# Last stage in two passes over the tokens, with the up projection in seven block products in place of eight

## The chip, the cores and the metric

The kernel runs on one core of one Trainium2 chip. Its engines work from queues of their own and meet at semaphores: TensorE (PE) multiplies 128x128 stationary blocks with up to 512 moving columns and writes to PSUM (8 banks of 512 fp32 columns); VectorE (DVE), ScalarE (ACT) and GpSimd (POOL) work elementwise; SyncE (SP) issues most DMAs, POOL the loads of the weights. The metric is the device time of one execution in microseconds (us), lower is better.

## The reference

All arrays are fp32. A linear attention with decay gives x of 3072 tokens by 512 features; an MLP with gate (F = 1536) and an MLP with SoLU and layer norm (F2 = 1024) follow.

```python
state = gamma * state + k_t v_t^T;  y_t = scale * q_t state      # 4 batches, 8 heads, 768 tokens
x = y as (3072, 512)
xn = x / sqrt(mean(x * x) + 1e-06) * rms_g
act = silu(xn @ w_gate) * (xn @ w_val)                            # (3072, 1536)
x2 = act @ w_out                                                  # (3072, 512), "down"
h = x2 @ w_in                                                     # (3072, 1024), "up"
e = exp(h - max(h));  solu = h * e / (sum(e) + 1e-09)
ln = (solu - mean(solu)) / sqrt(var(solu) + 1e-06) * g_ln
out = ln @ w_out2                                                 # (3072, 512), "down2"
```

## The kernel before

Each fp32 operand a of a large product is split in two parts, high (a rounded to fp32r, made by ACT) and low (a - high, made by DVE), and a product is three matmuls: high high, low high, high low (`split_products`, L282). The first stage (attention and gate and value products, up to about 562 us) is not touched; it leaves act in DRAM (`act_dram`) and has most weights split by then.

The last stage goes once over six tiles of 512 tokens (`tiles`, `stage_c`). Per tile:
- **down** (`down`, L571): for each of 12 blocks k of F, 4 x 3 matmuls into the banks 0 to 3 (`DOWN`). SP loads act block k (`load_act`), ACT makes `act_hi` (`act_high`, L744), DVE `act_lo` (`act_low`, L984), and PE waits for that one before step k. Four buffers of `act_hi` let ACT run up to four steps ahead.
- the four sums x2 are split from the banks to `x2_hi`, `x2_lo` in SBUF.
- **up** (`up`, L589): for each of four blocks of 128 tokens and each half of F2 (512 columns), 4 slices x 3 matmuls into one of the two banks `H`. ACT copies h, DVE takes the maximum (`row_max`), ACT the exponent, DVE normalises and centres (`softmax_h`, `centre`).
- **turn** (L602): four transposes into the bank `TURN`, twice per token block; ACT and DVE split the turned block. **down2** (L612): 12 matmuls, twice per token block, into the bank `Y2`. ACT scales and SP stores.

The order on each engine is written out by hand: down steps of tile t have turn and down2 of blocks 2 and 3 of tile t - 1 between them, and up products those of blocks 0 and 1.

Weights come in 26 pieces of 128x1024 through a buffer of three slots, `w_raw`. POOL may load piece m once the low part of piece m - 3 is made (`load_weights`, L450). ACT and DVE split a piece as `weights_high` (L694) and `weights_low` (L930); w_out2's pieces are first scaled by g_ln on DVE (`scale_weights`). In tile 0 the four pieces of w_in (18 to 21) are split behind act blocks 4 to 7, two of w_out2 behind blocks 8 and 9, the last two (24, 25) behind the sums.

## Time and profile before

| | |
|---|---|
| three runs, us | 1046.56, 1046.72, 1050.99 (median 1046.72) |
| profiled execution | span 1048.8 us; its time is given by that span alone, 2.1 us over the median of the runs |
| PE busy | 1023.9 us, 98% |
| DVE, ACT, POOL busy | 460.4, 431.9, 90.4 us |
| last stage | from 562.61 us to the end |
| matmuls in the profile | 5496 |

The profile is of one execution. "Busy" is the time in which an engine has an instruction running; PE's matmuls overlap, so the mean duration of one is more than the time from one start to the next. `[0.50 <-DVE solu L1047]` behind a row says that the engine was idle for 0.50 us before it and what released it.

### The profile page before, as it was taken

How to read it: one execution, taken by the hardware profiler on the slowest of the kernel's cores; microseconds unless marked ns; L12 is line 12 of the kernel's file. 1: busy time of each engine (PE TensorE's matmuls, PEld its weight loads, DVE VectorE, ACT ScalarE, POOL GpSimd, SP SyncE). 2: the span in 40 equal slices, each digit the busy share in tenths (PEclk: the TensorE clock that was granted, in tenths of full speed). 3: DMA queues.
4: the chain of work that ended last, by engine and by line, in shares of the span. 5: the costliest groups of instructions: out<-in, count | busy, mean ns of one | idle time of the engine just before them, and what ended most of it. 6: DMA issues, size and time to landing. Idle time of an engine off the chain costs nothing.

```text
span 1048.8 us, 15480 instructions
## 1 busy us (share of the span) xinstructions
PE 1023.9 (98%) x5496; PEld 900.6 (86%) x5496; DVE 460.4 (44%) x874; ACT 431.9 (41%) x776; POOL 90.4 (9%) x101
## 2 busy tenths in 40 slices
PE   6799999999998999999999999999999999999998
PEld 4489999999998999999999888888888888888886
DVE  3847635356352463433324653253253254244243
ACT  3445333243231442413223464364364264265255
POOL 5321110111001011100000000000000000000000
PEclk9999999999999999999999999999999999999999
DMA  7664331532314234313134403013012012012000
GB/s 229 210 217 146 106 108 52 166 114 93 119 46 138 98 113 136 111 51 120 66 115 135 137 21 101 1 60 100 0 60 90 10 60 90 10 60 91 11 21 31
DMA packets 75656, 95.51 MB, mean 91 GB/s; under 512 B 7248, under 2 KB 59728, under 8 KB 75600
## 3 DMA queue, kind: packets, MB, share of 16 engines
q1 hardware_dynamic: 71856, 81.11, 24.1%
q0 software_dynamic: 3744, 13.63, 3.9%
q8 instruction: 38, 0.62, 0.3%
q14 instruction: 18, 0.15, 0.0%
HBM read 64.04 MB, written 30.67 MB: 90 GB/s over the span
## 4 chain that ended last, share of the span: by engine, by line
PE 93%; DVE 2%; DMA 1%; ACT 1%; issue 1%; SPq 0%; POOL 0%; DVEq 0%; ACTq 0%; POOLq 0%
PE psum L284 28%; PE psum L286 28%; PE psum L285 27%; PE psum L521 3%; PE psum L531 3%; PE psum L609 2%; PE psum L513 1%; DMA w_raw<-weights 1%; PE psum L548 1%; DMA v_buf<-v_rows 0%; PE psum L501 0%; DVE w_gv_lo L936 0%; ACT L802 0%; DMA chunk_decay_t<-chunk_decay 0%; DVE probs L897 0%
## 5 line engine op out<-in xcount | busy, mean ns | idle before, releaser
L284 PE MATMUL psum<-xn_hi,w_gv_hi 128*128 128x384 f32 x768 | 267.1, 348 | 1.0 <-issue 1.0
L286 PE MATMUL psum<-xn_hi,w_gv_lo 128*128 128x384 f32 x768 | 258.4, 336 | 2.6 <-issue 2.6
L285 PE MATMUL psum<-xn_lo,w_gv_hi 128*128 128x384 f32 x768 | 257.7, 336 | 0.0
L764 ACT ACTIVATE silu<-psum 128x384 f32<-128x384 f32 x96 | 47.2, 492 | 283.6 <-PE psum L286 283.6
L284 PEld LDWEIGHTS psum<-xn_hi,w_gv_hi 128*128 128x128 f32 x768 | 145.2, 189 | 4.3 <-issue 3.4
L286 PEld LDWEIGHTS psum<-xn_hi,w_gv_lo 128*128 128x128 f32 x768 | 144.9, 189 | 2.9 <-issue 2.9
L285 PEld LDWEIGHTS psum<-xn_lo,w_gv_hi 128*128 128x128 f32 x768 | 145.3, 189 | 0.9
L998 DVE TENSOR_TENSOR act_buf<-psum,silu 128x384 f32<-128x384 f32 x96 | 53.5, 557 | 199.9 <-PE psum L286 116.7
L284 PE MATMUL psum<-act_hi,w_out_hi 128*128 128x512 f32 x288 | 114.2, 397 | 0.0
L286 PE MATMUL psum<-act_hi,w_out_lo 128*128 128x512 f32 x288 | 112.3, 390 | 0.0
L285 PE MATMUL psum<-act_lo,w_out_hi 128*128 128x512 f32 x288 | 112.3, 390 | 0.0
L464 POOL TENSOR_TENSOR q_dec<-kq_buf,q_decay_t 64x384 f32<-64x384 f32 x64 | 72.5, 1132 | 317.8 <-PE psum L531 210.4
L284 PE MATMUL psum<-w_out_hi,ln_t_hi 128*128 128x512 f32 x192 | 76.3, 398 | 0.4 <-ACT out_buf L827 0.4
L284 PE MATMUL psum<-w_in_hi,x_hi 128*128 128x512 f32 x192 | 76.1, 396 | 0.0
L286 PE MATMUL psum<-w_in_hi,x_lo 128*128 128x512 f32 x192 | 74.9, 390 | 0.0
L286 PE MATMUL psum<-w_out_hi,ln_t_lo 128*128 128x512 f32 x192 | 74.9, 390 | 0.0
L285 PE MATMUL psum<-w_out_lo,ln_t_hi 128*128 128x512 f32 x192 | 74.9, 390 | 0.0
L285 PE MATMUL psum<-w_in_lo,x_hi 128*128 128x512 f32 x192 | 74.8, 390 | 0.0
L897 DVE TENSOR_TENSOR probs<-psum,mask_t 128x256 f32<-128x256 f32 x96 | 40.1, 417 | 74.5 <-PE psum L286 52.2
L986 DVE TENSOR_TENSOR act_lo<-act_raw,act_hi 128x512 fp32r<-128x512 f32 x72 | 48.2, 689 | 55.4 <-ACT act_hi L753 55.4
L1026 DVE TENSOR_REDUCE neg_max<-h_buf 128x1 f32<-128x1024 f32 x24 | 29.3, 1220 | 93.6 <-ACT h_buf L798 93.5
L753 ACT ACTIVATE act_hi<-act_raw 128x512 fp32r<-128x512 f32 x72 | 43.8, 624 | 62.1 <-PE psum L286 53.8
(82 smaller groups left out, 1453.2 us busy)
## 6 DMA issues: line engine op xcount, KB each, us to landing
act_dram<-act_buf SPq DMA_DIRECT2D x96, 192.0 KB, 1.8
act_raw<-act_dram SPq DMA_DIRECT2D x72, 256.0 KB, 2.8
w_raw<-weights POOLq DMA_DIRECT2D x26, 512.0 KB, 4.9
kq_buf<-k_t SPq DMA_DIRECT2D x32, 192.0 KB, 2.8
kq_buf<-q_t SPq DMA_DIRECT2D x64, 96.0 KB, 2.9
k_buf<-k_rows SPq DMA_DIRECT2D x32, 192.0 KB, 2.9
v_buf<-v_rows SPq DMA_DIRECT2D x32, 192.0 KB, 3.1
out<-out_buf SPq DMA_DIRECT2D x24, 256.0 KB, 2.0
```

The lines of the kernel that those rows point to most:

```text
L284: pe.matmul(dst, w_hi, m_hi, start=start, stop=False)
L285: pe.matmul(dst, w_hi, m_lo, start=False, stop=False)
L286: return pe.matmul(dst, w_lo, m_hi, start=False, stop=stop)
L464: pool.tensor_tensor(q_dec[rows, r % 2, :, :], kq_buf[rows, q, :, (h + 1) * P:(h + 2) * P], q_decay_t[rows, q:q + 1, :].to_broadcast([HD, ...
L521: mm = pe.matmul(psum[h * HD:(h + 1) * HD, Y, 0:P], v_buf[:, q, i * P + h * HD:i * P + (h + 1) * HD], probs[:, ch % 2, h * P:(h + 1) * P], ...
L531: mm = pe.matmul(psum[:, Y, 0:P], state[:, q, (c - 1) % 2, :], q_dec[:, r % 2, i, :], start=False, stop=True, skip_group_check=True)
L753: act.activation(act_hi[:, k % 4, :], act_raw[:, k % 3, :], ACT.Copy).then_inc(act_hi_ready, 1)
L764: act.activation(silu[:, f % 2, :], psum[:, GATE[f % 2], 0:TB], ACT.Silu).then_inc(silu_ready, 1)
L897: dve.tensor_tensor(probs[:, ch % 2, :], psum[:, scores_bank(b, ch), 0:2 * P], mask_t[:, run_of(ch)[1], :], ALU.mult).then_inc(probs_ready, 1)
L986: dve.tensor_tensor(act_lo[:, k % 4, :], act_raw[:, k % 3, :], act_hi[:, k % 4, :].bitcast(F32), ALU.subtract).then_inc(act_lo_ready, 1)
L998: dve.tensor_tensor(act_buf[:, f % 3, :], psum[:, VALUE[f % 2], 0:TB], silu[:, f % 2, :], ALU.mult).then_inc(act_ready, 1)
L1026: dve.tensor_reduce(neg_max[:, j % 2:j % 2 + 1], h_buf[:, j % 2, :], AX_X, ALU.max, negate=True).then_inc(max_ready, 1)
```

## The change

The last stage becomes two passes. The first does the down steps of all six tiles one after the other and stores x2 to DRAM (`x_dram`). The second goes over twelve pairs of token blocks (256 tokens), loads x2 of the pair, and does up, turn and down2. For a pair, the up projection is a 2x2 block product: rows the two token blocks, columns the two halves of F2, and the inner dimension in two halves of 256. It is done by the Winograd form of Strassen's scheme in seven block products of 6 matmuls each: three operands of x2 are plain blocks (A11, A12, A22), four are sums and differences that POOL makes (S1 to S4); three of the weights are plain (B11, B21, B22), four are differences that DVE makes in the raw buffer (T1 to T4). Sums of products are formed by accumulating in the banks PX, PY, PV, by two copies of a bank on ACT (`copy_xy`, `copy_p7`) and two additions on DVE (`sum_u3`, `sum_c22`). turn and down2 of the pair before stand between the products. All pieces of w_out2 are now split in tile 0.

```diff
@@ tensor
+            def product(half, bank, a, b, start):
+                dst = psum[:, bank, :]
+                for kc in range(HK):
+                    pe.matmul(dst, xa_hi[half][:, a, kc, :], w_in2_hi[:, b, kc, :], start=start and kc == 0, stop=False, ...)
+                    pe.matmul(dst, xa_hi[half][:, a, kc, :], w_in2_lo[:, b, kc, :], start=False, stop=False, ...)
+                    mm = pe.matmul(dst, xa_lo[half][:, a, kc, :], w_in2_hi[:, b, kc, :], start=False, stop=kc == HK - 1, ...)
+                return mm
+            def pair(n, half, before):
+                pe.wait_ge(xa_lo_ready, 3 * (n + 1))
+                if before:
+                    pe.wait_ge(h_copied, 3 * n - 2)
+                product(half, PX, A11, B11, True).then_inc(p1_done, 1)
+                if before:
+                    pe.wait_ge(h_copied, 3 * n - 1)
+                product(half, PV, S3, T3, True).then_inc(p7_done, 1)
+                if before:
+                    turn(n - 1, 1, 0)
+                pe.wait_ge(xy_copied, n + 1)
+                product(half, PY, S2, T2, False).then_inc(p6_done, 1)
+                product(half, PX, A12, B21, False).then_inc(c11_done, 1)
+                if before:
+                    turn(n - 1, 1, 1)
+                    down2(n - 1, 1, 0)
+                pe.wait_ge(u3_ready, n + 1)
+                product(half, PY, S1, T1, False).then_inc(p5_done, 1)
+                if before:
+                    turn(n - 1, 0, 0)
+                    down2(n - 1, 1, 1)
+                product(half, PV, A22, T4, False).then_inc(c21_done, 1)
+                if before:
+                    turn(n - 1, 0, 1)
+                pe.wait_ge(c22_ready, n + 1)
+                product(half, PY, S4, B22, False).then_inc(c12_done, 1)
+                if before:
+                    down2(n - 1, 0, 0)
+                    down2(n - 1, 0, 1)
+            tiles(pe, down_tile)
+            tiles(pe, up_tile)
@@ scalar
+            def down_tile(t, first, last):
                 for k in range(4, FC):
                     act_high(t, k)
-                    if first and k < 10:
-                        weights_high(WI2_PIECE + k - 4)
+                    if first and k in (4, 6):
+                        in2_base_high((k - 4) // 2)      # waits for both pieces of the half
+                    if first and k in (5, 7):
+                        in2_t_high((k - 5) // 2)         # waits for the four differences
+                    if first and k >= 8:
+                        weights_high(WO2_PIECE + k - 8)
+                if not last:
+                    for k in range(3):
+                        act_high(t + 1, k)
+                copy_x2(t, 0)
+                copy_x2(t, 2)
+                if not last:
+                    act_high(t + 1, 3)
+                else:
+                    operands_high(0, 0)
@@ vector
+            def in2_t(half):
+                one, two = in2_slots(half)
+                b11, b12, b21, b22 = one[:, 0, :], one[:, 1, :], two[:, 0, :], two[:, 1, :]
+                dve.wait_ge(wi2_base_lo, 2 * half + 2)
+                dve.tensor_tensor(b11, b12, b11, ALU.subtract).then_inc(wi2_t_made, 1)
+                dve.tensor_tensor(b12, b22, b12, ALU.subtract).then_inc(wi2_t_made, 1)
+                dve.wait_ge(wi2_t_made, 4 * half + 2)
+                dve.tensor_tensor(b22, b22, b11, ALU.subtract).then_inc(wi2_t_made, 1)
+                dve.wait_ge(wi2_t_made, 4 * half + 3)
+                dve.tensor_tensor(b21, b21, b22, ALU.subtract).then_inc(wi2_t_made, 1)
+            def down_tile(t, first, last):
                 for k in range(4, FC):
                     act_low(t, k)
+                    if first and k in (4, 6):
+                        in2_base_low((k - 4) // 2)
+                        in2_t((k - 4) // 2)
+                    if first and k in (5, 7):
+                        in2_t_low((k - 5) // 2)          # frees the two raw slots
+                    if first and k >= 8:
+                        weights_low(WO2_PIECE + k - 8)
+                if not last:
+                    for k in range(3):
+                        act_low(t + 1, k)
+                copy_x2(t, 1)
+                copy_x2(t, 3)
+                if not last:
+                    act_low(t + 1, 3)
+                else:
+                    operands_low(0, 0)
+            def pair(n, half, before, more):
...
+                sum_u3(n)                                # bank PV = bank PY + p7_buf
...
+                if more:
+                    operands_low(n + 1, 1 - half)
+                sum_c22(n)                               # h_buf = bank PY + p7_buf
...
+                row_max(n, 1)
+                row_max(n, 0)
+                for j in (1, 0):
+                    softmax_h(n, j)
+                    centre(n, j)
@@ gpsimd
+            def sums(n):
+                pool.wait_ge(x2_loaded, DMA * (n + 1))
+                at_least(pool, xa_lo_ready, 3 * n)
+                pool.tensor_tensor(s3, x2_blocks(first, 0), x2_blocks(first, 1), ALU.subtract).then_inc(s_made, 1)
+                pool.tensor_tensor(s1, x2_blocks(first, 1), x2_blocks(second, 1), ALU.add).then_inc(s_made, 1)
+                pool.tensor_tensor(s2, s1, x2_blocks(first, 0), ALU.subtract).then_inc(s_made, 1)
+                pool.tensor_tensor(s4, x2_blocks(second, 0), s2, ALU.subtract).then_inc(s_made, 1)
@@ sync
+            def load_x2(n, tiles_stored):
+                at_least(sp, xa_lo_ready, 3 * n)
+                for d in range(KC):
+                    sp.wait_ge(x2_stored[d], DMA * tiles_stored)
+                sp.dma_start(x2_raw[:], x_dram[:, :, bass.ds(n * 2 * P, 2 * P)] ...).then_inc(x2_loaded, DMA)
```

In the order of instructions, DVE's queue in tile 0 of the last stage, before, from the low part of act block 4 on (`w_in_lo`, `w_out_lo` are low parts of weight pieces):

```order
L986 TENSOR_TENSOR act_lo<-act_raw,act_hi 128x512
L936 TENSOR_TENSOR w_in_lo<-w_raw,w_in_hi 128x1024
L986 TENSOR_TENSOR act_lo<-act_raw,act_hi 128x512
L936 TENSOR_TENSOR w_in_lo<-w_raw,w_in_hi 128x1024
L986 TENSOR_TENSOR act_lo<-act_raw,act_hi 128x512
```

The same queue after the change, from the low part of act block 6 on (the second half of w_in):

```order
L1126 TENSOR_TENSOR act_lo<-act_raw,act_hi 128x512
L1168 TENSOR_TENSOR w_in_lo<-w_raw,w_in_hi 128x512
L1171 TENSOR_TENSOR w_in_lo<-w_raw,w_in_hi 128x2x512
L1179 TENSOR_TENSOR w_raw<-w_raw 128x512
L1180 TENSOR_TENSOR w_raw<-w_raw 128x512
L1182 TENSOR_TENSOR w_raw<-w_raw 128x512
L1184 TENSOR_TENSOR w_raw<-w_raw 128x512
L1126 TENSOR_TENSOR act_lo<-act_raw,act_hi 128x512
L1190 TENSOR_TENSOR w_in_lo<-w_raw,w_in_hi 128x2x512
L1193 TENSOR_TENSOR w_in_lo<-w_raw,w_in_hi 128x2x512
L1126 TENSOR_TENSOR act_lo<-act_raw,act_hi 128x512
```

Between the low parts of two act blocks there was one instruction; now there are six and two by turns. ACT's queue after the change, from the high part of act block 6 on:

```order
L853 ACTIVATE act_hi<-act_raw 128x512
L900 ACTIVATE w_in_hi<-w_raw 128x512
L901 ACTIVATE w_in_hi<-w_raw 128x2x512
L853 ACTIVATE act_hi<-act_raw 128x512
L907 ACTIVATE w_in_hi<-w_raw 128x2x512
L908 ACTIVATE w_in_hi<-w_raw 128x2x512
L853 ACTIVATE act_hi<-act_raw 128x512
```

The high part of act block 7 stands behind those of the plain blocks, which need the fourth piece of w_in. Last, DVE's queue after the change where the passes meet, from the last two copies of x2 on:

```order
L1162 COPY x_out<-psum 128x512 x2
L1199 TENSOR_TENSOR xa_lo<-x_raw,xa_hi 128x512
L1204 TENSOR_TENSOR xa_lo<-x_raw,xa_hi 128x256
L1207 TENSOR_TENSOR xa_lo<-s_raw,xa_hi 128x1024
L1216 TENSOR_TENSOR psum<-psum,p_buf 128x512
L1199 TENSOR_TENSOR xa_lo<-x_raw,xa_hi 128x512
L1204 TENSOR_TENSOR xa_lo<-x_raw,xa_hi 128x256
L1207 TENSOR_TENSOR xa_lo<-s_raw,xa_hi 128x1024
L1221 TENSOR_TENSOR h_buf<-psum,p_buf 128x512
L1227 TENSOR_REDUCE neg_max<-h_buf 128x1 x2
```

The operands of pair 0 (`xa_lo`) stand behind the copies of the last sums, and those of pair 1 ahead of the second addition of pair 0 (L1221).

## Rows read from the trace of the kernel before

**Rows 1.** The page, busy us (share of the span) xinstructions
```profile
PE 1023.9 (98%) x5496; PEld 900.6 (86%) x5496; DVE 460.4 (44%) x874; ACT 431.9 (41%) x776; POOL 90.4 (9%) x101
```

**Rows 2.** By stretch: us, busy us (x instructions), PEclk the granted clock
```profile
550.00:600.00 50.00, 50.00 (x239) 43.57 (x238) 25.14 (x36) 19.28 (x28) 3.17 (x6) 1.00 0.44 143
...
900.00:950.00 50.00, 50.00 (x229) 41.33 (x228) 19.76 (x36) 24.67 (x39) 0.00 (x0) 1.00 0.10 32
```

**Rows 3.** What PE waited for in the last stage: us, times, longest
```profile
PE psum L609 <- DVE solu L1047: 0.5, 1, 0.5
PE psum L609 <- DVE ln_t_lo L1052: 0.4, 1, 0.4
PE psum L284 <- ACT out_buf L827: 0.4, 1, 0.4
```

**Rows 4.** PE timeline, last stage: start us, us, line, out<-in
```profile
562.61 0.39 PE L284 MATMUL psum<-act_hi,w_out_hi 128*128 128x512 f32 x1
...
566.05 0.39 PE L284 MATMUL psum<-act_hi,w_out_hi 128*128 128x512 f32 x1
...
584.41 0.39 PE L284 MATMUL psum<-act_hi,w_out_hi 128*128 128x512 f32 x1
```

**Rows 5.** PE by line, last stage: busy us, mean ns
```profile
L285 PE MATMUL psum<-w_in_lo,x_hi 128*128 128x512 f32 x192 | 74.8, 390 | 0.0
```

**Rows 6.** ACT timeline, first down tile
```profile
568.68 1.21 ACT L753 ACTIVATE act_hi<-act_raw 128x512 fp32r<-128x512 f32 x2 [6.94 <-DMA act_raw<-act_dram]
...
578.67 1.06 ACT L698 ACTIVATE w_in_hi<-w_raw 128x1024 fp32r<-128x1024 f32 x1 [2.71 <-DMA w_raw<-weights]
```

**Rows 7.** DVE timeline, first down tile
```profile
569.34 1.29 DVE L986 TENSOR_TENSOR act_lo<-act_raw,act_hi 128x512 fp32r<-128x512 f32 x2 [5.32 <-ACT act_hi L753]
...
580.90 0.69 DVE L986 TENSOR_TENSOR act_lo<-act_raw,act_hi 128x512 fp32r<-128x512 f32 x1
...
584.76 0.69 DVE L986 TENSOR_TENSOR act_lo<-act_raw,act_hi 128x512 fp32r<-128x512 f32 x1
```

**Rows 8.** POOL timeline: the loads of weight pieces
```profile
572.40 0.53 POOL L453 DMA_DIRECT2D w_raw<-weights  x1 [11.18 <-DVE w_in_lo L936]
```

**Rows 9.** ACT and DVE by line, last stage: busy us, mean ns
```profile
L698 ACT ACTIVATE w_in_hi<-w_raw 128x1024 fp32r<-128x1024 f32 x4 | 4.2, 1051 | 2.7 <-DMA w_raw<-weights 2.7
...
L936 DVE TENSOR_TENSOR w_in_lo<-w_raw,w_in_hi 128x1024 fp32r<-128x1024 f32 x4 | 4.9, 1224 | 3.3 <-ACT w_in_hi L698 3.3
```

**Rows 10.** Page and DMA list: issues, KB each, median us to landing
```profile
act_raw<-act_dram SPq DMA_DIRECT2D x72, 256.0 KB, 2.8
w_raw<-weights POOLq DMA_DIRECT2D x26, 512.0 KB, 4.9
...
out<-out_buf SPq DMA_DIRECT2D x24, 256.0 KB, 2.0
...
x_tile<-x_dram SPq DMA_DIRECT2D x7, 768.0 KB, 4.7
```

**Rows 11.** DVE and POOL timelines, where both work
```profile
125.11 1.41 DVE L904 TENSOR_TENSOR kq_lo<-kq_buf,kq_hi 128x384 fp32r<-128x384 f32 x1
...
128.41 0.56 DVE L904 TENSOR_TENSOR kq_lo<-kq_buf,kq_hi 128x384 fp32r<-128x384 f32 x1
...
125.09 2.31 POOL L464 TENSOR_TENSOR q_dec<-kq_buf,q_decay_t 64x384 f32<-64x384 f32 x2 [7.82 <-PE psum L531]
```

**Rows 12.** ACT and PE timelines, first h to first transpose
```profile
600.93 0.60 ACT L798 ACTIVATE h_buf<-psum 128x512 f32<-128x512 f32 x1 [0.74 <-PE psum L286]
...
606.83 0.66 PE L609 MATMUL psum<-ident,solu 128*128 128x128 f32 x4 [0.50 <-DVE solu L1047]
```

**Rows 13.** PE timeline and stretches after a pause in the first stage
```profile
327.77 0.44 PE L286 MATMUL psum<-xn_hi,w_gv_lo 128*128 128x384 f32 x1 [2.58 <-issue]
...
329.00:330.00 1.00, 1.00 (x5) 1.00 (x4) 0.00 (x0) 0.00 (x0) 0.00 (x0) 0.50 0.92 233
...
332.00:333.00 1.00, 1.00 (x6) 1.00 (x6) 0.00 (x0) 0.00 (x0) 0.71 (x1) 0.79 0.59 150
```

More of the change, by code:

```diff
@@ L98, in retention_moe_kernel @@
     GROUPS = 4 * FC
+    OPERANDS, HK = 7, KC // 2
+    A11, A12, A22, S3, S2, S1, S4 = range(OPERANDS)
+    B11, B21, B22, T1, T3, T4, T2 = range(OPERANDS)
+    PAIRS_C = B * S // (2 * P)
+    WI2_ROWS = (0, 2, 1, 3)
     def steps_at(*ranges):
@@ new lines, in _, with up_tile @@
+            pe.wait_ge(w_lo_ready, WI2_PIECE)
+            pe.wait_ge(rms_ready, B_TILES)
+            pe.wait_ge(y_copied, B * BC)
+            pe.wait_ge(probs_ready, B * BC)
+            pe.wait_ge(state_ready, 2 * B * BKV)
+            def down_tile(t, first, last):
+                for k in range(FC):
+                    down(t, k)
+            def up_tile(t, first, last):
+                for half in range(2):
+                    pair(2 * t + half, half, not (first and half == 0))
+            tiles(pe, down_tile)
@@ new lines, in copy_x2, with in2_base_high @@
+                act.activation(x2_out[:, d, :], psum[:, DOWN[d], :], ACT.Copy).then_inc(x2_act_copied, 1)
+            def in2_base_high(half):
+                for i in range(2):
+                    m = WI2_PIECE + 2 * half + i
+                    act.wait_ge(w_loaded[m % RAW], DMA * (m // RAW + 1))
+                one, two = in2_slots(half)
+                act.activation(w_in2_hi[:, B11, half, :], one[:, 0, :], ACT.Copy).then_inc(wi2_base_hi, 1)
+                act.activation(w_in2_hi[:, B21:B22 + 1, half, :], two, ACT.Copy).then_inc(wi2_base_hi, 1)
@@ new lines, in up_tile @@
+            def up_tile(t, first, last):
+                for half in range(2):
+                    pair(2 * t + half, half, not (first and half == 0), not (last and half == 1))
+            tiles(act, down_tile)
+            act.wait_ge(w_lo_ready, PIECES)
+            tiles(act, up_tile)
+            n = PAIRS_C - 1
+            ln_high(n, 1, 0)
+            ln_high(n, 1, 1)
+            deviation(n, 1)
+            ln_high(n, 0, 0)
+            scale_out(n, 1)
+            ln_high(n, 0, 1)
@@ new lines, in in2_t @@
+            def in2_t(half):
+                one, two = in2_slots(half)
+                b11, b12, b21, b22 = one[:, 0, :], one[:, 1, :], two[:, 0, :], two[:, 1, :]
[6 more added lines that the diff above has]
+                dve.tensor_tensor(b21, b21, b22, ALU.subtract).then_inc(wi2_t_made, 1)
@@ new lines, in pair @@
+            def pair(n, half, before, more):
+                if before:
+                    ln_low(n - 1, 1, 0)
+                sum_u3(n)
+                if before:
+                    ln_low(n - 1, 1, 1)
+                    invert_deviation(n - 1, 1)
+                if more:
+                    operands_low(n + 1, 1 - half)
+                sum_c22(n)
+                if before:
+                    ln_low(n - 1, 0, 0)
+                    invert_deviation(n - 1, 0)
+                    ln_low(n - 1, 0, 1)
+                row_max(n, 1)
+                row_max(n, 0)
+                for j in (1, 0):
+                    softmax_h(n, j)
+                    centre(n, j)
@@ L1112, with up_tile @@
+            def up_tile(t, first, last):
+                for half in range(2):
+                    pair(2 * t + half, half, not (first and half == 0), not (last and half == 1))
+            tiles(dve, down_tile)
+            tiles(dve, up_tile)
+            n = PAIRS_C - 1
+            ln_low(n, 1, 0)
+            ln_low(n, 1, 1)
+            invert_deviation(n, 1)
+            ln_low(n, 0, 0)
+            ln_low(n, 0, 1)
+            invert_deviation(n, 0)
 def kernel(**inputs):
```

502 lines of the change are left out of this document (254 added, 248 removed).

## The prediction

> **What bounds the kernel now.** I read the page's busy shares first, then the busy time by stretch, then what TensorE waited for in the last stage, then its timeline. TensorE (PE) is busy 98% of the span [rows 1], and in the last stage, from 562.61 us on, it is busy for the whole of 50 us stretches at granted clock 1.00, the 2.4 GHz level, while ACT has 19 to 25 and DVE 20 to 25 of each 50 us [rows 2]. In the 486 us of that stage it waits three times, 1.3 us together [rows 3]. So a matmul taken out there is worth its full issue interval, and whatever ACT or DVE is late by is lost in full. The mean of a matmul in the list (390 ns) is not its price, since matmuls overlap: from 566.05 to 584.41 us 81 of them start in 18.36 us, one per 0.227 us [rows 4]. A step k of the down projection (12 matmuls) is 2.72 us.
>
> **What is removed.** The up projection has three groups of 192 matmuls [rows 5], 576 in all: per pair of token blocks 2 blocks x 2 halves x 4 slices x 3 split products = 48. Seven products of 2 slices x 3 are 42. Twelve pairs save 72 matmuls, 72 x 0.227 = 16.3 us. Transposes (48 groups of four) and the down2 products keep their number. The order shows this on PE; nothing of it is in doubt.
>
> **What is added beside it, part one: the first down tile.** The weights of the up projection are now seven operands: for each half, ACT and DVE split three plain blocks, DVE makes four differences in place in the raw buffer, ACT and DVE split those too, and only then is the raw slot free for the next load. All of this stands in ACT's and DVE's queues between the splits of act block k, on which PE's step k waits; step k is due at 562.61 + 2.72k.
> - Until 570.6 DVE is where it was: act_lo 3 and 4 done [rows 7]. Durations: 1024 columns take ACT 1.05 and DVE 1.22 [rows 9], 512 take 0.60 [rows 12] and 0.69 [rows 7], some 0.1 less when they follow each other.
> - First half: ACT from 569.8 [rows 6] makes both plain parts by 571.4; DVE's large low part ends at 572.6; four differences (priced as the DVE row of 512 columns, each behind the one before) 2.7 us, to 575.3; act_lo 5 at 575.9, due 576.2: just in time. ACT's two parts of the differences 575.3 to 577.3, DVE's low parts 577.6 and 578.7, act_lo 6 at 579.3, due 578.9: PE idle 0.5 us.
> - Fourth quarter of the weights: its slot is free at 577.6, where before POOL sent it off at 572.40 [rows 8]. Before, ACT got it at 578.67 after a 2.71 us wait [rows 6], 6.3 us from issue; the median of all 26 loads is 4.9 [rows 10]. I take 5.5: it lands at 583.2. ACT waits with the splits of this half in front of act block 7, which queues behind it. ACT to 584.8, DVE's low part 585.9, differences 588.6, act_lo 7 at 589.3. PE wanted it at 582.1: idle 7.3 us.
> - Step 8: DVE first does the two low parts of the differences (to 592.0), then act_lo 8 at 592.7: 0.8 us late.
> - Steps 9, 10, 11: between two of them DVE scales a w_out piece, waits for ACT's high part, makes the low part and then act_lo. The trace has this very loop: act_lo at 580.90 and 584.76, 3.86 us [rows 7]. Before, two pieces went through it with steps in stock; now four do with none: 3 x (3.86 - 2.72) = 3.4 us.
> - Into tile 1: behind act_lo 11 DVE has the last piece (3.2 us), three act_lo (1.8) and only then the copy of the second sum bank (0.7), 5.7 us; PE wants that bank 3.5 us after act_lo 11. 2.2 us.
> Sum for the first tile: 0.5 + 7.3 + 0.8 + 3.4 + 2.2 = 14.2 us. In tiles 1 to 5 ACT and DVE have one split per 2.72 us and the copies of a bank end about 1 us before PE comes back to it: nothing.
>
> **Part two: the change of passes.** Before, the first up product followed its sums with stored work; its only wait, 0.50 us at the first transpose [rows 3], goes. Now, with E the last down tile's end:
> - DVE copies the last bank (to E + 0.9), then splits pair 0's operands: 0.6, 0.4 and 1.2 us. First product at E + 3.3: idle 3.3 us, nothing lies beside it.
> - Pair 0 has no transposes or down2 between its products, so PE runs six in 8.2 us and is at the seventh at E + 11.5. It waits for DVE's second sum, which stands behind the splits of pair 1. Those need: last store (256 KB, 2.0 us), load of 512 KB (between the 2.8 us of 256 KB and the 4.7 of 768 KB: 4.0) [rows 10], landed E + 7.3; four POOL operations of 128x256 (the trace has 1.16 us for 64x384 [rows 11], two thirds of it: 0.75 each) to E + 10.3; ACT's 1.05, DVE's 1.2 and the sum's 0.7: E + 13.3. Idle 1.9 us.
> - The seventh product ends at E + 14.9. From the second copy of h to the first transpose the trace takes 5.9 us (600.93 to 606.83, through maximum, table load, exponent, normalising, centring) [rows 12]; one more maximum and POOL beside it make 6.4: E + 21.3. PE has two products until E + 17.4. Idle 3.9 us.
> Sum 9.1 us. From pair 1 on down2 and transposes fill: a pair takes PE 90 x 0.227 + 4 x 0.44 = 22.2 us. ACT's part: 0.49 of its time now [rows 2] is 40 us of an 81 us tile, less 12 act splits (7.5) and 4 of the x2 splits is 15 us a pair, plus two bank copies and three operand splits (3.3): 18 of 22 us, in an order in which each piece is asked for after at least one further product. I take 0; the closest is the copy of the first product, with under 1 us to spare.
>
> **Part three: the tail.** The two blocks of the last pair now come out of the products together. The first transpose waits 0.6 us for the centring, and the second (same bank) for a low part that queues on DVE behind the other block's normalising: 2.8, where the trace has 0.4 [rows 3]. The difference is 0.6 + 2.8 - 0.4, less some 0.6 that the later wait gives back: +2.4.
>
> **Clock.** After 2.58 us without a matmul the granted clock was at 0.50 (1.2 GHz) from about 1.3 us after the restart at 327.77 until it was mixed again in the stretch at 332, some 3.4 us [rows 13]; at half speed that stretch loses 1.7 us. Behind the 7.3 us idle time such a stretch is covered by the waits of steps 8 and 9. Between the 3.3, 1.9 and 3.9 us I count one that is not: +1.6; bounds 0 and 4.8 (one after each and in the tail).
>
> **The sum.** -16.3 + 14.2 - 0.5 + 9.1 + 2.4 + 1.6 = +10.5 us. The profiled span of 1048.8 becomes 1059.3; the runs' median is 1046.7, so 1057.2 us.
>
> Unknown costs and their ends: the load, immediate (-4.5) to 6.3 us (+0.8); the POOL operations 0.5 to 1.4 us each (-0.5 to +3.1), nearest row 1.16 for more columns; the copy from bank to bank and the sum into a bank, which no row shows, as the ACT and DVE rows of 512 columns or twice that (0 to +3); differences in place -0.5 to +1. Together about -6 to +8, seldom all on one side.
>
> A rule against the change: two DVE rows stand beside POOL's work at 125.09, where DVE's two-input operation of 384 columns took 1.41 us instead of 0.56 [rows 11]. The Trainium skill, GPSIMD Engine Reference, "Key points", says that GpSimd shares its SBUF interfaces with VectorE and collides with DVE instructions that have two SBUF inputs; the trace agrees. By that rule, were each of the four operations of a pair to hold DVE up once by 0.85 us, a pair would put 3.4 us more on DVE, against 0 if none did.
>
> **Rivals.**
> - *The splits are hidden.* If ACT and DVE had act block 7 ready in spite of the 11 more instructions, the first tile would lose nothing: -16.3 + 9.1 - 0.5 + 2.4 = -5.3, 1041.4 us. For it: ACT has a pause of 2.71 us there now [rows 6]. Against it: that chain is 7.3 us too long, and even an immediate fourth load leaves 2.8 of it. It decides where act_lo 7 comes before 582. A middle case, load soon and no slow clock, gives +4: 1051.
> - *The clock falls after every pause*, in the tail too: +3.2 more, 1060.4 us. The pause of 2.58 us speaks for it, since three of the new ones are longer; the waits of steps 8 to 11 and of the tail, which would hide a part, speak against it.
> - *The pairs wait.* The product copy's spare time is under 1 us; 0.5 us a pair for eleven pairs, from POOL's contention or a slow bank copy, is +5.5: 1062.7 us. Against it: DVE's 0.40 of its time now [rows 2], 32 us of a tile, less 16 splits of 0.69, is 10.5 us a pair, plus 3.7 for sums and operands: 14 of 22 us.
> - *No fewer matmuls* can be excluded by the order.
>
> **Chances.** A change under 0.5%, 5.2 us, can't be told from none. Forecast 0.63 (its own range 1053 to 1060), hidden splits 0.06, middle case 0.08, clock 0.14, waiting pairs 0.09. Faster 0.05, same 0.10 (the middle case and the edge of the hidden one), slower 0.85. Range 1050 to 1064: it leaves out the hidden case and the ends.
>
> **What would show it.** PE: 72 fewer matmuls; an idle time of about 7 us before step 7 of the first down tile, smaller ones to its end; idle about 3, 2 and 4 us within 25 us of the change of passes; none above 0.5 us in pairs 2 to 11; granted clock 0.50 for 3 us at two places. ACT waits about 5 us for the fourth quarter of w_in. I am wrong if act_lo 7 is ready when step 7 is due, or if the pairs lose time in the loop.

## The result, and the profile after

| | before | after |
|---|---|---|
| median, us (range, runs) | 1049.68 (1046.56 to 1053.99, 5) | 1064.06 (1056.46 to 1066.37, 5) |
| ratio | | 1.0124, 95% interval 1.0081 to 1.0167 |
| profiled execution, span | 1048.8 | 1054.7 |
| last stage: its start, its length | 562.61, 486.2 | 557.87, 496.8 |
| matmuls in the profile | 5496 | 5424 |

The change makes the kernel slower by 1.2%. The forecast was 1057.2 us with a range of 1050 to 1064 and slower at 0.85, so the median of 1064.06 stands right on the upper edge of the range. Of the 6.9 us between forecast and median, 3.0 are the kernel before, whose median is 1049.68 us over five runs where the forecast started from 1046.72 over three. As a ratio the forecast was 1.0100, which lies in the interval. The last stage is 10.6 us longer; the forecast's sum was +10.5. The spans don't show that by themselves, because the stages ahead of it, whose code is the same, took 562.6 us in one execution and 557.9 in the other. So the terms are read from the length of the last stage (first `w_out_hi` matmul to the end of the span).

The page of the changed kernel, answering [rows 1] (busy us, share of the span, xinstructions):

```profile
PE 1014.1 (96%) x5424; PEld 888.7 (84%) x5424; DVE 504.6 (48%) x934; ACT 443.4 (42%) x804; POOL 126.5 (12%) x149
```

TensorE does less and is busy for a smaller share: 98% has become 96%. What it waited for in the last stage, answering the three rows of [rows 3] (us, times, longest):

```profile
PE psum L317 <- DVE act_lo L1126: 7.5, 5, 5.5
PE psum L699 <- DVE e_buf L1247: 4.1, 2, 3.6
PE psum L684 <- DVE xa_lo L1207: 3.1, 1, 3.1
PE psum L699 <- DVE ln_t_lo L1253: 2.6, 1, 2.6
PE psum L684 <- DVE h_buf L1221: 1.6, 1, 1.6
PE psum L317 <- ACT x_out L892: 1.0, 1, 1.0
PE psum L317 <- DVE x_out L1162: 0.7, 1, 0.7
PE psum L317 <- ACT out_buf L963: 0.4, 1, 0.4
```

21.0 us where there were 1.3. Where they stand, in PE's timeline (start us, us, line, out<-in, idle before it and its releaser):

```profile
583.15 0.79 PE L317 MATMUL psum<-act_hi,w_out_hi 128*128 128x512 f32 x1 [5.51 <-DVE act_lo L1126]
...
590.48 0.50 PE L317 MATMUL psum<-act_hi,w_out_hi 128*128 128x512 f32 x1 [0.23 <-DVE act_lo L1126]
...
594.33 0.50 PE L317 MATMUL psum<-act_hi,w_out_hi 128*128 128x512 f32 x1 [0.83 <-DVE act_lo L1126]
...
602.13 0.50 PE L317 MATMUL psum<-act_hi,w_out_hi 128*128 128x512 f32 x1 [0.97 <-ACT x_out L892]
...
769.70 0.47 PE L684 MATMUL psum<-w_in_hi,xa_hi 128*128 128x512 f32 x1 [3.13 <-DVE xa_lo L1207]
...
781.35 0.50 PE L684 MATMUL psum<-w_in_hi,xa_hi 128*128 128x512 f32 x1 [1.60 <-DVE h_buf L1221]
...
789.37 0.66 PE L699 MATMUL psum<-ident,e_buf 128*128 128x128 f32 x4 [3.61 <-DVE e_buf L1247]
```

There are two clusters and a tail: the first down tile and the first step of tile 1 (557.87 to about 604), the change of passes, and the last pair (its waits of 0.5 and 2.6 us are in the table above and not in these rows). Between 790 us and the last pair no row of a wait is left.

The starts of all matmuls and transposes of the last stage give the whole account. From the first start to the last it is 482.62 us before and 493.26 after, +10.6. Of that: 72 matmuls fewer at 0.228 us, -16.4; starts more than 0.6 us after the one before, +21.1 (the interval less 0.228 us, against the same sum in the kernel before); starts in stretches of granted clock 0.50, +4.2; the rest (waits under 0.6 us, and matmul after transpose), +1.7.

### The profile page after: what moved, and what is told of

Read it like the earlier page. It is cut to its first block, busy times and chain, and to the rows that moved or that the text cites. A ratio compares the mean times of both kernels' runs of the same rounds, so it can differ in the third digit from the quotient of the medians.

```text
span 1054.7 us, 15828 instructions
## 1 busy us (share of the span) xinstructions
PE 1014.1 (96%) x5424; PEld 888.7 (84%) x5424; DVE 504.6 (48%) x934; ACT 443.4 (42%) x804; POOL 126.5 (12%) x149
## 4 chain that ended last, share of the span: by engine, by line
PE 89%; DVE 6%; ACT 2%; issue 2%; DMA 1%; SPq 0%; POOL 0%; ACTq 0%; DVEq 0%; POOLq 0%
PE psum L317 23%; PE psum L319 22%; PE psum L318 22%; PE psum L684 4%; PE psum L688 4%; PE psum L686 4%; PE psum L615 3%; PE psum L625 3%; PE psum L699 2%; PE psum L607 2%; PE psum L595 1%; DVE w_gv_lo L1076 0%; DVE w_out_lo L1076 0%; PE psum L642 0%; DVE e_buf L1237 0%
## 5 line engine op out<-in xcount | busy, mean ns | idle before, releaser
L317 PEld LDWEIGHTS psum<-act_hi,w_out_hi 128*128 128x128 f32 x288 | 54.4, 189 | 23.1 <-DVE act_lo L1126 9.7
L684 PE MATMUL psum<-w_in_hi,xa_hi 128*128 128x512 f32 x168 | 68.6, 408 | 4.7 <-DVE xa_lo L1207 3.1
L1253 DVE TENSOR_TENSOR ln_t_lo<-psum,ln_t_hi 128x512 fp32r<-128x512 f32 x48 | 33.1, 689 | 74.5 <-ACT ln_t_hi L945 74.5
L688 PE MATMUL psum<-w_in_hi,xa_lo 128*128 128x512 f32 x168 | 66.3, 394 | 0.0
```

The costliest lines, as they stand in the source:

```text
L317: pe.matmul(dst, w_hi, m_hi, start=start, stop=False)
L684: pe.matmul(dst, xa_hi[half][:, a, kc, :], w_in2_hi[:, b, kc, :], start=start and kc == 0, stop=False, skip_group_check=True)
L688: mm = pe.matmul(dst, xa_lo[half][:, a, kc, :], w_in2_hi[:, b, kc, :], start=False, stop=kc == HK - 1, skip_group_check=True)
```

## The experiments

Each ran beside the kernel before, on one chip for each group. Three groups shared their runs of before: medians 1051.92 (19 runs; `again`, `filler`, `spread`, `all`), 1050.0 (29 runs; `eighth`, `gates`, `place`, `best`) and 1051.83 us (15 runs; `switch`, `best2`).

| kernel | median us | ratio to before, 95% interval | last stage, us | PE's waits in it, us | lost at 0.50 clock, us |
|---|---|---|---|---|---|
| before | | | 486.2 | 1.3 | 0.0 |
| after | 1064.06 | 1.0124 (1.0081 to 1.0167) | 496.8 | 21.0 | 4.2 |
| again | 1063.23 | 1.0116 (1.0091 to 1.0141) | 496.9 | 21.0 | 4.4 |
| filler | 1061.08 | 1.0076 (1.0046 to 1.0107) | 495.2 | 12.9 | 1.1 |
| eighth | 1080.06 | 1.0268 (1.0229 to 1.0307) | 517.0 | 20.7 | 8.4 |
| switch | 1057.98 | 1.0066 (1.0043 to 1.0090) | 494.6 | 17.7 | 6.0 |
| spread | 1059.87 | 1.0073 (1.0052 to 1.0095) | 496.6 | 19.4 | 6.7 |
| gates | 1053.12 | 1.0023 (1.0000 to 1.0045) | 486.4 | 13.0 | 3.1 |
| place | 1053.77 | 1.0021 (0.9995 to 1.0047) | 489.6 | 13.3 | 6.1 |
| all | 1050.06 | 0.9987 (0.9969 to 1.0005) | 486.2 | 11.9 | 4.0 |
| best | 1046.39 | 0.9965 (0.9942 to 0.9988) | 480.2 | 8.7 | 1.7 |
| best2 | 1040.79 | 0.9906 (0.9881 to 0.9930) | 476.6 | 5.8 | 1.2 |

The last column is the sum, over matmuls that start in a stretch of granted clock 0.50 or up to 0.25 us ahead of it, of the interval to the next start less 0.2275 us, without intervals over 0.6 us. The last three columns are of one profiled execution each, and the medians of all runs. For `after`, `best`, `gates` and `all` the profiled one was among the fastest (1056.46 us where the median is 1064.06, 1040.31 for 1046.39, 1049.06 for 1053.12, 1046.17 for 1050.06), so a size is surest where both agree.

**`again`**: the changed kernel once more.

> The changed kernel itself, unchanged, for its granted clock. Its profiled execution (1056.5 us, clock 0.993) had three stretches of 3.4 us at 1.2 GHz in the last stage, the other four (1063 to 1066 us) a mean clock of 0.982 to 0.984. Theory A (each pause of PE in the last stage can drop the clock, and in most executions more of them do): again 1063 to 1066 us with a clock of 0.982 to 0.985 in most runs, and the kernel before at 0.993 or more. Theory B (the spread comes from the first stage, which is the same in both): the kernel before shows the same spread of clocks and times.

The last stage came out as 496.9 against 496.8 us and the waits as 21.0 both times, with three half-clock stretches of 3.4 us at the same three places, while the stage started at 566.87 instead of 557.87 us. So the 9 us between these two executions lie in the stages ahead of it, as theory B has it. Its other half holds too: the 19 runs of the kernel before spread over 8.3 us (1046.52 to 1054.84) with clocks of 0.990 to 0.998. Part of theory A stays: the six runs of the changed kernel had clocks of 0.982 to 0.987, all below those.

**`filler`**: matmuls into an unread bank where TensorE waits.

```
+            def filler(w, n):
+                for _ in range(n):
+                    pe.matmul(psum[:, 1, :], w[:, 0:P], w[:, 0:BANK], start=True, stop=True)
...
+                    if first and k == 7:
+                        filler(w_out_hi, 20)
...
+            filler(w_out2_hi, 11)
...
+            filler(w_out2_hi, 9)
```

> The changed kernel with idle matmuls of 512 columns into a bank nobody reads: 20 ahead of step 7 of the first down tile, 11 between the passes, 9 between the last pair's first two transposes (40 x 0.227 = 9.1 us of PE work, all in pauses of 5.5, 3.1 and 2.6 us). What the other engines wait for is the same. Theory A (clock): no stretch at 1.2 GHz at these places, so 2 x 1.7 us less against the profiled execution and more against the others: 1050 to 1055 us, clock 0.99. Rival (the pauses cost only themselves, clock plays no part): the same as the changed kernel within 1 us, or up to 1 us more for fillers that outlast a pause.

The loss at half clock fell from 4.2 to 1.1 us and one stretch was left, where the wait of 3.7 us for the first transpose had no filler. The other runs agree: over eight runs the mean granted clock was 0.986 to 0.997, where `again` had 0.982 to 0.987. But the median, 1061.08 us, is well above the 1050 to 1055 expected. In `filler` (waits of PE in the last stage):

```profile
PE psum L704 <- DVE e_buf L1256: 4.2, 2, 3.7
PE psum L317 <- DVE act_lo L1135: 3.9, 6, 0.8
```

The stage became only 1.6 us shorter. In tile 0 six waits for `act_lo` add up to 3.9 us, where the changed kernel had 2.0 in its four smaller ones: steps 8 to 11 come at the period of DVE's queue, so that a step done sooner is waited out behind it. Measured by starts, tile 0 lost 12.3 us here and 12.5 in the changed kernel: the 1.5 us of half clock in it had been covered by DVE's queue. What the fillers gained lies mainly at the switch (1.6) and in the tail (1.1), and the stretch behind the unfilled wait took 1.1 back.

**`eighth`**: an eighth product in each pair. It is summed twice, so this kernel's output is not the reference's; it is for its time alone.

```
-                product(half, PX, A12, B21, False).then_inc(c11_done, 1)
+                product(half, PX, A12, B21, False)
+                product(half, PX, A12, B21, False).then_inc(c11_done, 1)
```

> The changed kernel with an eighth block product of 6 matmuls in each of the 12 pairs (A12 times B21 is summed twice, so the output is not the reference's), nothing else moved. Theory: the last stage is bound by TensorE in all pairs but the first two, so 72 matmuls at 0.227 us come back whole: last stage 496.8 + 16.3 = 513 us, median about 1079 against 1063 for the changed kernel. Rival: the pairs are bound by the vector engines' chain of copies and softmax, TensorE fills pauses that the records hide, and the eighth product costs under 8 us: last stage under 505 us.

The ratio rose from 1.0116 to 1.0268, 0.0152 or 16.0 us. In the profile the stage is 20.2 us longer, 4 more than expected: 16.4 for 72 matmuls, 4.2 for half clock (five stretches beside matmuls instead of three), and waits as in the changed kernel. Both are above the 8 us of the rival. So the 16 us that seven products save against eight are gained in full; what ate them stands elsewhere.

**`switch`**: the pass switch alone.

```
                 if not last:
                     for k in range(3):
                         act_high(t + 1, k)
+                else:
+                    operands_high(0, 0)
                 copy_x2(t, 0)
                 copy_x2(t, 2)
...
                     load_x2(0, 1)
+                    load_x2(1, 1)
                 store_x2(t)
```

(The same for `operands_low` on DVE; pair 0's copy and PV product wait for the last copies of the first pass.)

> The changed kernel with the pass switch alone reordered: ScalarE and VectorE make the operands of pair 0 ahead of the last tile's copies, and SyncE loads pair 1 ahead of the last tile's stores. Theory: of the three pauses at the switch (3.13, 1.60 and 3.61 us) the first goes, as it was ScalarE's and VectorE's order of work, and the other two stay, as they are pair 0's chain of sums and softmax with no older pair behind it: last stage 493-495 us (496.8 less 3), tile 0's 12 us unchanged. Rival: pair 0's operands wait for the load and sums of GpSimd and not for the order, and the first pause stays over 2.5 us: last stage 496-498 us.

PE's waits in the last stage of `switch`:

```profile
PE psum L317 <- DVE act_lo L1131: 7.3, 4, 5.5
PE psum L700 <- DVE e_buf L1252: 4.2, 2, 3.7
PE psum L700 <- DVE ln_t_lo L1258: 2.6, 1, 2.6
PE psum L685 <- DVE h_buf L1226: 1.6, 1, 1.6
```

The row for `xa_lo` is gone, the others stand as they were, and the stage is 494.6 us: as expected. The 3.1 us were the order of ACT's and DVE's queues. The stage is only 2.2 us shorter, because 1.8 us more went at half clock. Part of that isn't the edit's: tile 0 has the code of the changed kernel and nearly its waits (5.5, 0.8, 0.8, 0.9 and 0.7 us, here without the one of 0.2), yet the clock was at 0.50 for 6.8 us there and not 3.4, and once more behind the last of these waits (us, busy us of PE, PEld, DVE, ACT, POOL, then the granted clock, DMA share, GB/s):

```profile
611.00:613.00 2.00, 2.00 (x6) 1.62 (x5) 0.00 (x0) 0.00 (x0) 0.00 (x0) 0.50 1.06 407
```

`eighth` had the same two stretches there. So two executions of the same code and waits can differ by about 1.5 us in this stage.

**`spread`**: fewer splits in the first down tile. The second half of w_in went to its steps 9 and 10, the four w_out2 pieces to the last tile.

```
-                    if first and k in (4, 6):
-                        in2_base_low((k - 4) // 2)
+                    if first and k in (4, 9):
+                        in2_base_low((k - 4) // 5)
...
-                    if first and k >= 8:
-                        weights_low(WO2_PIECE + k - 8)
+                    if last and k in (4, 6, 8, 10):
+                        weights_low(WO2_PIECE + (k - 4) // 2)
```

> The splits of the first down tile spread out: the second half of w_in behind act blocks 9 and 10 of the first tile, the four pieces of w_out2 behind blocks 4, 6, 8, 10 of the last tile. Forecast's theory (the first tile's queue costs 13 to 14 us in the sum, 10 in the profile): the pauses of 5.5, 0.2, 0.8, 0.8 us in that tile go, 1.1 us at most stays, so 9 to 11 us less than the changed kernel, 1046 to 1055 us. Rival (PE would lose the same time elsewhere, as ACT and DVE have too much to do in the first pass): no gain, pauses in the last tile instead.

It failed: the waits of the tile went from 9.2 to 7.6 us and the stage stayed at 496.6; the median, 1059.87, is above the 1046 to 1055 expected. ACT's timeline in `spread` shows why:

```profile
585.37 0.63 ACT L853 ACTIVATE act_hi<-act_raw 128x512 fp32r<-128x512 f32 x1 [7.31 <-DMA act_raw<-act_dram]
...
602.02 0.63 ACT L853 ACTIVATE act_hi<-act_raw 128x512 fp32r<-128x512 f32 x1 [6.57 <-DMA act_raw<-act_dram]
602.56 1.07 ACT L892 ACTIVATE x_out<-psum 128x512 f32<-128x512 f32 x2
```

ACT was no longer behind with work; it waited for the hidden layer itself, 7.31 and 6.57 us, and with it the copy L892 that PE's next tile needs. GpSimd sends two weight loads off ahead of each of these waits, as soon as slots are free:

```profile
576.84 0.53 POOL L529 DMA_DIRECT2D w_raw<-weights  x1 [16.67 <-DVE w_in_lo L1190]
577.97 0.53 POOL L529 DMA_DIRECT2D w_raw<-weights  x1 [0.60 <-DVE w_in_lo L1193]
...
594.16 0.53 POOL L529 DMA_DIRECT2D w_raw<-weights  x1 [15.65 <-DVE w_in_lo L1190]
595.29 0.53 POOL L529 DMA_DIRECT2D w_raw<-weights  x1 [0.61 <-DVE w_in_lo L1193]
```

The loads of act that were in flight with them took up to 7.0 us to land (issued at 578.31, 578.91 and 579.52 us: 7.0, 6.9 and 6.9), where the median of the kernel is 2.8.

**`gates`**: `spread` with three of those loads held back.

```
                     for m in range(WO_PIECE, PIECES):
+                        if m > WO2_PIECE - 1 and m < PIECES - 1:
+                            pool.wait_ge(act_lo_ready, FC * (m - WO2_PIECE + 2))
                         load_weights(m)
```

> The kernel `spread` (second half of the up weights at steps 9 and 10 of tile 0, w_out2 in the last tile), with one edit: GpSimd issues the loads of three w_out2 pieces only in tiles 1, 2 and 3, so that none is in flight together with another in tile 0. Theory: in `spread` two weight loads of 512 KB in flight held the loads of the hidden layer for up to 7.3 us, and ScalarE waited for these: the wait of TensorE for ScalarE's copy L892 ahead of tile 1 falls from 4.5 us to under 1.5 us and the last stage from 496.6 to 487-491 us, median about 1053-1055. Rival: the wait of 4.5 us is the work of ScalarE and VectorE themselves (the loads are late because their buffer slots come free late): it stays over 3 us and the last stage at 495 us or more.

The stage fell by 10.2 us, from 496.6 to 486.4, and ACT's longest waits in this stretch were 4.05 us and 2.84:

```profile
581.61 0.63 ACT L855 ACTIVATE act_hi<-act_raw 128x512 fp32r<-128x512 f32 x1 [4.05 <-DMA act_raw<-act_dram]
...
594.54 0.63 ACT L855 ACTIVATE act_hi<-act_raw 128x512 fp32r<-128x512 f32 x1 [2.84 <-DMA act_raw<-act_dram]
```

The same three loads of act landed in 3.9 to 4.0 us, beside one weight load. PE's wait for that copy fell from 4.5 to 0.8 us. The amount of splitting is the same; what differs is how many 512 KB loads are in flight beside the 256 KB ones. This is what hid the gain of `spread`. The stage is 0.6 us shorter than expected. Its size is less sure than the cause: of the 10.2 us, 6.4 are waits and 3.6 half clock, and over all runs the ratios differ by 0.0050, or 5.3 us, each with an interval of 2 us and more to either side. The Trainium skill, DMA: Bandwidth & Descriptors, "Issuing engines are not separate DMA queues", says that transfers from different engines' queues run on the same 16 DMA engines and interleave; the trace agrees: moving GpSimd's loads changed when SyncE's landed.

**`all`**: `spread`, `switch`, and three edits more: in pair 0 the second sum ahead of the operands of pair 1 (and ACT's two bank copies of pair 1 beside the exponents of pair 0), in pair 1 four products ahead of the first transpose, in the tail a split ahead of the last centring.

> Everything that the reading of the trace suggests: the splits spread out as in the run before; operands of pair 0 split ahead of the last copies of x2, pair 1 (it lies in tile 0) loaded ahead of the last stores; second sum of pair 0 ahead of the operands of pair 1; in pair 1 four products ahead of the first transpose; in the last pair one low part ahead of the other block's normalising. Forecast's theory: PE's idle time in the last stage falls from 21 us to about 7, and with 16.3 us of matmuls gone the kernel comes out 9 to 11 us ahead of the kernel before: about 1037 to 1040 us. Rival (the saving of the seven products isn't there, since two passes cost PE something in the pairs): not faster than the kernel before.

It missed: 1050.06 us where 1037 to 1040 was expected, with a stage of 486.2 us, as long as before's. Its waits are those of `spread` at the first tile (ACT x_out 4.1 us, act_lo 2.4), and 3.9 us for `ln_t_lo`. The first two are what `gates` later gave back.

**`place`**: the splits elsewhere, and two of GpSimd's loads held back to match; the rest as in the changed kernel.

```
+                    if (first and k == 6) or (last and k == 4):
+                        in2_base_low(0 if first else 1)
+                        in2_t(0 if first else 1)
+                    if (first and k == 7) or (last and k == 5):
+                        in2_t_low(0 if first else 1)
+                    if last and k in (7, 8, 10, 11):
+                        weights_low(WO2_PIECE + (7, 8, 10, 11).index(k))
```

> The changed kernel with the splits of the up weights put elsewhere and nothing else: the first half at steps 6 and 7 of tile 0, the second half at steps 4 and 5 of the last tile, the four w_out2 pieces at steps 7, 8, 10 and 11 of the last tile, GpSimd's loads apart from each other. Theory: tile 0's loss of 12 us goes whole, no wait over 1 us is left in the first pass; the switch and the tail stay: last stage 481-485 us (496.8 less 12 to 15), median 1048-1051, ratio to before about 1.00. Rival: the splits' work comes back in the last tile, as the stock of steps cannot take it at either place: last stage over 490 us.

One wait of 0.5 us is left in the first pass, so tile 0's waits went whole, and the ratio fell from 1.0124 to 1.0021. This shows that the placing of the splits and of their loads made tile 0's loss. But the stage is 489.6 us, neither the 481 to 485 of the theory nor the rival's 490 and more: the switch now costs 4.0 us in its first wait (splits stand at steps 10 and 11 ahead of it; `best2` tests this), and 6.1 us went at half clock instead of 4.2. Two of its stretches (columns as above):

```profile
764.00:769.00 5.00, 4.44 (x11) 3.50 (x12) 0.42 (x1) 0.58 (x1) 0.00 (x0) 0.50 0.64 209
...
785.00:789.00 4.00, 3.81 (x11) 3.23 (x12) 3.26 (x9) 2.64 (x4) 0.00 (x0) 0.50 0.00 0
```

At the switch the clock was at 0.50 twice for 6.8 us, where the changed kernel had it once for 3.4.

**`best`**: `place` with the edits of `switch` and `all`.

> `place` together with what `all` had for the switch of passes and the tail (operands of pair 0 ahead of the copies of the last tile, pair 1 loaded ahead of the stores, four products of pair 1 ahead of the first transpose, second sum of pair 0 ahead of pair 1's operands, first split of the tail ahead of the last block's centring). Theory: tile 0's loss, most of the switch's and 1 us of the tail's go together, and the 72 matmuls less are then gained: last stage 473-478 us against 486.2 of the kernel before, median 1038-1043, ratio 0.987 to 0.992. Rival: the waits come back elsewhere as in `all`: last stage 484 us or more, ratio over 0.996.

The stage is 480.2 us and the ratio 0.9965 (0.9942 to 0.9988): faster than before, with 1 just outside the interval, and short of the 473 to 478 us and 0.987 to 0.992 expected. The wait for pair 0's operands was 2.8 us and not gone.

**`best2`**: `best` with the second half of w_in at steps 6 and 7 of tile 1, and w_out2 at steps 4, 5, 7 and 9 of the last tile, with four of GpSimd's loads held back to match.

> `best` with the splits placed again: the second half of the up weights at steps 6 and 7 of tile 1, the four w_out2 pieces at steps 4, 5, 7 and 9 of the last tile, so that nothing but the operands stands ahead of the pass switch. Theory: the 2.8 us wait ahead of pair 0 in `best` was made by splits at steps 10 and 11: it falls under 1 us, and with it the stretch at 1.2 GHz there; last stage 476-479 us against 480.2 in `best` and 486.2 before, ratio 0.991 to 0.995. Rival: the 2.8 us is the chain load, GpSimd's sums and operands of pair 0 whatever stands ahead of it: the wait stays over 2 us, last stage 479-481 us.

PE's waits in its last stage:

```profile
PE psum L711 <- DVE ln_t_lo L1280: 4.3, 2, 2.8
PE psum L696 <- ACT psum L941: 0.6, 1, 0.6
PE psum L711 <- DVE e_buf L1274: 0.5, 1, 0.5
```

(A fourth, of 0.4 us for `out_buf`, is in the kernel before too.) No wait is left in the first pass or ahead of pair 0: the 2.8 us of `best` went when the splits left the last steps. The stage is 476.6 us, 9.6 less than before and as expected, and the ratio 0.9906 (0.9881 to 0.9930), a little better than the 0.991 to 0.995 expected. It is faster than both kernels: the seven products do pay when their weights are prepared where the queues have room.

## Why the prediction was right, step by step

| step | forecast, us | measured, us | from |
|---|---|---|---|
| 72 matmuls | -16.3 | -16.4 | starts; `eighth` |
| first tile, until the second sum of tile 1 starts | +14.2 | +12.5 | PE timeline |
| before's 0.5 at the first transpose | -0.5 | -0.5 | [rows 3] |
| switch: 3.3 + 1.9 + 3.9 | +9.1 | 3.13 + 1.60 + 3.61 = +8.3 | PE timeline |
| tail | +2.4 | 0.5 + 2.6 - 0.4 = +2.7 | waits after less [rows 3] |
| clock outside tile 0 | +1.6 | 1.6 + 1.1 = +2.7 | starts |
| sum | +10.5 | 10.6 in the stage (these rows: 9.3) | |

- **Saving.** Right, and `eighth` shows it by itself.
- **First tile.** The mechanism is the one forecast, 1.7 us smaller. The differences took 0.68 and 0.69 us each as priced (the first, in DVE's timeline of the changed kernel):

```profile
567.72 0.69 DVE L1179 TENSOR_TENSOR w_raw<-w_raw 128x512 f32<-128x512 f32 x1
```

The term that was mis-sized is the fourth quarter's load: issued at 573.12 us and in ACT's hands at 576.88, 3.8 us where I took 5.5.

```profile
573.12 0.53 POOL L529 DMA_DIRECT2D w_raw<-weights  x1 [16.63 <-DVE w_in_lo L1190]
```

```profile
576.88 0.63 ACT L900 ACTIVATE w_in_hi<-w_raw 128x512 fp32r<-128x512 f32 x1 [3.85 <-DMA w_raw<-weights]
...
582.53 1.06 ACT L907 ACTIVATE w_in_hi<-w_raw 128x1024 fp32r<-128x1024 f32 x1 [3.55 <-DVE w_raw L1184]
```

So step 7 waited 5.5 us and not 7.3. Step 8 waited 0.23 us and not 0.8, because step 7 itself ran in part at half clock and so reached it later. The loop of steps 8 to 11 has the period taken from [rows 7]: act_lo starts at 585.89, 589.74, 593.59 and 597.40 us, 3.85 apart (3.81 the last).
- **Switch.** All three waits came where forecast and within 0.3 us. `switch` removed the first by order alone. The durations that the prediction lists for it (0.9, 0.6, 0.4 and 1.2 us) add up to 3.1 and not 3.3, which is what it measured.
- **Tail.** As forecast, 0.5 and 2.6 us where 0.6 and 2.8 were expected; the 0.6 that I let a later wait give back did not show in the waits.
- **Pairs.** The rival "the pairs wait" is out: no wait between 790 us and the last pair. By stretch, as in [rows 2], ACT is busy for 0.71 of the time, 15.8 us of a pair's 22.2 where 18 was forecast, and DVE for 0.60, 13.4 us where 14 was:

```profile
900.00:950.00 50.00, 50.00 (x240) 41.26 (x239) 30.21 (x56) 35.68 (x60) 6.47 (x9) 1.00 0.17 58
```

- **Clock.** Mis-sized by 1.1 us. The rival "the clock falls after every pause" had part of the truth: half clock came with the wait of 5.5 us, after 3.1 and after the tail's 2.6, though not after the pauses of 1.6 and 3.6. The losses were 1.5, 1.6 and 1.1 us. The first was covered, as forecast: `filler` had no such stretch in tile 0, and the tile came out only 0.2 us shorter. The other two are 2.7 us where I had 1.6. `filler`, in which the stretches went where the pauses were filled, shows that the pauses bring it. The stretch after 582, the one after 770 and the one in the tail:

```profile
582.00:583.00 1.00, 0.00 (x0) 0.00 (x0) 1.00 (x2) 0.47 (x1) 0.00 (x0) 0.84 0.00 0
...
770.00:773.00 3.00, 3.00 (x9) 2.38 (x8) 0.00 (x0) 0.58 (x1) 0.00 (x0) 0.57 0.61 176
...
1037.00:1039.00 2.00, 2.00 (x8) 1.71 (x8) 0.43 (x1) 1.06 (x2) 0.00 (x0) 0.50 0.00 0
```

So the sum of +10.5 against 10.6 owes something to luck: tile 0 and the switch were 2.5 us too dear, the clock and the tail 1.4 too cheap, and 1.3 us is in no step. Some 0.5 of it is at the switch, where the intervals between starts exceed the usual one by 8.8 us and the idle times add up to 8.3; the rest stays open. The mechanism was not luck: the waits came at the places forecast, and `place`, `switch` and `eighth` each moved one term by itself.
- **GpSimd beside DVE.** The rule weighed in the prediction cost nothing in the loop of pairs, where GpSimd's sums took their 0.72 to 0.75 us each. DVE's instructions of this time read PSUM (POOL, then DVE, of the changed kernel):

```profile
883.38 0.74 POOL L574 TENSOR_TENSOR s_raw<-s_raw,x_raw 128x256 f32<-128x256 f32 x1
```

```profile
883.94 0.69 DVE L1253 TENSOR_TENSOR ln_t_lo<-psum,ln_t_hi 128x512 fp32r<-128x512 f32 x1 [2.24 <-ACT ln_t_hi L945]
```

At the change of passes it did cost. At the end of the first pass, where PE did not wait for it, one of pair 0's sums took 1.17 us and two `act_lo` beside them 1.18 and 1.24 for 0.69. Then the last of pair 2's sums fell beside the normalising (DVE, 1.28 us by itself), which stands in the chain to the first transpose, and held it up by 0.4 of the 3.61 us that PE waited there (the other 23 of this instruction took 1.28 or 1.29 us):

```profile
786.52 0.72 POOL L576 TENSOR_TENSOR s_raw<-x_raw,s_raw 128x256 f32<-128x256 f32 x1
```

```profile
786.63 1.70 DVE L1237 SCALAR_TENSOR_TENSOR e_buf<-h_buf,e_inv,e_buf 128x1024 f32<-128x1024 f32 x1
...
789.61 1.28 DVE L1237 SCALAR_TENSOR_TENSOR e_buf<-h_buf,e_inv,e_buf 128x1024 f32<-128x1024 f32 x1
```

In `best` the first sums fell beside DVE's splits, which have two SBUF inputs, and there both were held up (POOL 1.75 for 0.74, DVE's act_lo 1.23 for 0.69):

```profile
749.50 1.75 POOL L575 TENSOR_TENSOR s_raw<-x_raw 128x256 f32<-128x256 f32 x1
```

```profile
747.77 0.48 DVE L1083 TENSOR_SCALAR w_raw<-w_raw,ln_g_col 128x512 f32<-128x512 f32 x1
...
750.58 1.23 DVE L1141 TENSOR_TENSOR act_lo<-act_raw,act_hi 128x512 fp32r<-128x512 f32 x1
751.73 1.84 DVE L1083 TENSOR_SCALAR w_raw<-w_raw,ln_g_col 128x512 f32<-128x512 f32 x2
```

The Trainium skill, GPSIMD Engine Reference, "Key points", names DVE instructions in a 2-port perf mode or with two SBUF inputs as the ones that collide; both traces agree with that for two inputs. The last row shows that one wide input can be enough: two scalings of a w_out2 piece beside the sums took 1.84 us together, where one by itself took 0.48. Whether these run in such a mode no row tells. This stood ahead of pair 0 in `best`, and may be a part of its 2.8 us; it was not tried apart.

**Left open.** The ratios say 12 to 13 us (1.0116 and 1.0124 of 1050), the last stage 10.6; the interval of the ratio, 9 to 18 us, holds it. The medians of `again` and of the 19 runs beside it are 11.3 us apart, which leaves 0.6 us for the stages ahead. Their length varied more than that between executions: the last stage started at 557.9 to 566.9 us, with 3.4 us of half clock ahead of it in the first case and 20.5 us in the other. Why was not tried.

## What to carry to other kernels

Work taken off an engine that was busy 98% of the time was worth its full issue interval here, but the gain shows only if the work that the scheme adds on the other engines is placed where their queues have room. The same seven products made this kernel 1.2% slower with all weight preparation in one tile. They left it as it was (1.0021) with the preparation elsewhere, and made it 0.9% faster with that over three tiles and the order at the switch and in the tail mended too. When a split is spread out, spread its loads too: a load that goes off as soon as a slot is free can delay the one that is needed next. Count a wait of 3 us on TensorE as dearer than its length where no other wait follows to cover it: in the changed kernel two such waits brought 1.6 and 1.1 us more at half clock.

## What the runs showed of the hardware that was not expected

- Loads of 256 KB took up to 7.0 us to land with two 512 KB loads of another queue in flight (`spread`), and 4.0 in the same place with one (`gates`), against a median of 2.8. One can be enough, though: in `best2` a load of act issued at 582.98 us took 6.3 beside a single weight load. Keeping them apart was worth 10.2 us of the profiled stage and 5.3 by the ratios (`gates` against `spread`).
- Half clock (granted 0.50, the 1.2 GHz level) came in pieces of 3.4 or 6.8 us, and not by the length of the wait alone. It came behind waits of 5.5, 4.0, 3.1, 2.6 and 2.4 us (the last in `all`), and in `switch` and `eighth` behind a run of waits of 1.0 us at most. It did not come after 3.6 us at the switch in the changed kernel, nor after 2.6 in the tail of `switch`, while `filler` had it after 3.7. The same wait of about 5.4 us in the same code had 3.4 us of it in two executions and 6.8 in two others.
- GpSimd's sums and DVE's work held each other up where DVE's instruction read wide tensors from SBUF alone: 1.75 us for 0.74 on GpSimd, 1.23 for 0.69 on DVE with two of them (1.70 for 1.28 on DVE alone in the changed kernel), and 1.84 for two instructions of 0.48 with one. But a maximum over `h_buf` beside them took 1.22 us, where the others took 1.21, and `ln_t_lo`, read from PSUM, kept its 0.69.
